# Output-weight remainders on VectorE, one block sum moved ahead of the moments, and tensor-and-scalar forms for 128x1 operations in an attention, experts and SoLU kernel

## The reference, cut to what matters

```python
def _moe_ref(x, domain_probs, w1, w2):
    for e in range(E):                       # 4 experts, 512 -> 1024 -> 512
        h = np.maximum(x @ w1[e], 0.0)
        out += p[:, e:e + 1] * (h @ w2[e])

def _moe2_ref(x, w_in, w_out, g_ln):
    h = x @ w_in                             # 1536 x 512 @ 512 x 1024
    h_max = np.max(h, axis=-1, keepdims=True)
    e = np.exp(h - h_max)
    sm = e / (np.sum(e, axis=-1, keepdims=True) + 1e-09)
    solu = h * sm
    mu = np.mean(solu, axis=-1, keepdims=True)
    var = np.mean((solu - mu) ** 2, axis=-1, keepdims=True)
    ln = (solu - mu) / np.sqrt(var + 1e-06) * g_ln
    return (ln @ w_out).astype(np.float32)   # 1536 x 1024 @ 1024 x 512
```

## Time and profile before

| what | value |
|---|---|
| median of 3 runs | 753.34 us (753.29 to 753.89) |
| the profiled execution's own time | 753.5 us |
| its span, first to last instruction | 751.7 us |
| mean granted clock of PE | 1.000 |
| PE busy | 744.6 us, 99% |
| DVE busy | 525.5 us, 70% |
| POOL busy | 341.0 us, 45% |
| ACT busy | 218.9 us, 29% |

### The profile page before, as it was taken

One profiled execution on the slowest core, in us unless ns is written; L12 is line 12 of the kernel. 1 busy time (PEld: TensorE's weight loads), 2 busy tenths in 40 slices (PEclk: granted clock), 3 DMA queues, 4 the chain that ended last, 5 costly groups with the idle time before them and its releaser, 6 DMA issues. The chain is left out here.

```text
span 751.7 us, 12616 instructions
## 1 busy us (share of the span) xinstructions
PE 744.6 (99%) x3994; PEld 652.9 (87%) x3994; DVE 525.5 (70%) x1042; ACT 218.9 (29%) x414; POOL 341.0 (45%) x326
## 2 busy tenths in 40 slices
PE   9999999999999999999999999999999999999998
PEld 8888899899898998989988898898898877888876
DVE  5677767676666766767666676676767799867772
ACT  5677641111111111111211112111113743433332
POOL 4367546253542535425354253543535974442400
PEclk9999999999999999999999999999999999999999
DMA  9756310100101000010000100000022100000001
GB/s 263 194 142 167 105 31 2 56 29 29 31 26 56 28 28 28 28 56 28 28 28 28 56 28 28 28 28 0 1 112 66 49 0 15 15 29 28 16 28 42
DMA packets 39106, 37.15 MB, mean 49 GB/s; under 512 B 14497, under 2 KB 31905, under 8 KB 39073
## 3 DMA queue, kind: packets, MB, share of 16 engines
q1 hardware_dynamic: 37472, 34.64, 15.0%
q10 hardware_dynamic: 1600, 2.10, 0.8%
HBM read 33.59 MB, written 3.15 MB: 49 GB/s over the span
## 5 line engine op out<-in xcount | busy, mean ns | idle before, releaser
L809 PE MATMUL y_ps<-w2s,hs 128*128 128x512 f32 x1140 | 286.0, 395 | 0.1
L789 PE MATMUL p_ps<-xs,ws 128*128 128x384 f32 x1344 | 255.2, 336 | 0.0
L809 PEld LDWEIGHTS y_ps<-w2s,hs 128*128 128x128 f32 x1140 | 212.4, 188 | 41.0 <-DVE acc L1474 0.6
L789 PEld LDWEIGHTS p_ps<-xs,ws 128*128 128x128 f32 x1344 | 237.6, 188 | 11.0
L1474 DVE SCALAR_TENSOR_TENSOR acc<-y_ps,pr,acc 128x512 f32<-128x512 f32 x178 | 133.0, 748 | 79.6 <-PE y_ps L809 78.6
L1121 ACT ACTIVATE hs<-hs_sum 128x384 fp32r<-128x384 f32 x128 | 67.4, 527 | 353.6 <-DVE hs_sum L1442 238.9
L1461 DVE SCALAR_TENSOR_TENSOR hs<-hs_sum,hs 128x384 fp32r<-128x384 f32 x128 | 93.2, 737 | 4.3 <-ACT hs L1121 2.2
L577 POOL TENSOR_TENSOR ws_sum<-raw_sum 128x256 f32<-128x256 f32 x16 | 11.8, 739 | 146.8 <-PE p_ps L789 146.0
L608 POOL CAST w2s<-raw_sum 128x1024 fp32r<-128x1024 f32 x16 | 16.9, 1056 | 86.1 <-PE y_ps L809 86.1
L1134 ACT ACTIVATE neg_s<-neg_s,row 128x256 f32<-128x256 f32 (+1 forms) x96 | 42.2, 483 | 26.0 <-DVE row L1493 25.9
L1493 DVE CUSTOM_DVE_ANT_0 neg_s<-s_ps,bias 128x256 f32<-128x256 f32 (+1 forms) x96 | 34.3, 399 | 20.2 <-PE s_ps L823 18.1
(11 more groups left out here) (152 smaller groups left out, 971.2 us busy)
## 6 DMA issues: line engine op xcount, KB each, us to landing
raw_sum<-in_w SPq DMA_DIRECT2D x28, 512.0 KB, 3.5
qk<-in_qkW SPq DMA_DIRECT2D x24, 256.0 KB, 3.7
qk<-in_qkW SPq DMA_DIRECT2D x24, 128.0 KB, 4.1
v_sb<-in_v SPq DMA_DIRECT2D x16, 192.0 KB, 3.0
out<-o_sb SPq DMA_DIRECT2D x12, 256.0 KB, 2.0
raw_sum<-in_w ACTq DMA_DIRECT2D x4, 512.0 KB, 7.0
raw_sum<-in_w_in SPq DMA_DIRECT2D x1, 2048.0 KB, 8.0
wout_lo_a_sum<-in_w_out SPq DMA_DIRECT2D x1, 1792.0 KB, 7.6
```

The costliest lines, as they stand in the source:

```text
L789: mm = nc.tensor.matmul(bank, ws[slot][:, w, part, kk, :], xs[:, 2 * bt + kk, x, part, :], start=(kk == 0 and w == 1 and x == 1), stop=(kk ...
L809: mm = nc.tensor.matmul(mixed_at(s, t), hs[bt][:, h, b, tok], w2s[slot][:, w, f, :], start=(f == 0 and h == 1 and w == 1), stop=(f == 1 an ...
```

## The change

- `w_out`: ACT no longer scales chunks 0 to 3 in place. The high parts of all eight chunks are made with the gain as scale, those of chunks 0 to 3 where the scaling stood. POOL's `split_wout` is gone. DVE makes all eight remainders: chunk 0 inside step 31, chunks 1 to 3 behind the last `add_up`s, chunks 4 to 7 one by one between the first block sums.
- `w_in`: POOL makes six remainders instead of five, DVE one instead of two.
- DVE's loop over steps ends one round (four steps) earlier, and that round is written out.
- In the second pair `late_left(1)` stands ahead of `moments(0)`.
- Five 128x1 operations of DVE (`largest`, one in `moments`, two in `normal`) take the form with one tensor and one scalar per partition.

```diff
-    WIN_POOL = 5
+    WIN_POOL = 6
...
-            def split_wout(c):
-                pool.wait_ge(wouthi_ready, c + 1)
-                pool.sem_inc(pool_waited, 1)
-                nc.gpsimd.tensor_tensor(wout_lo(c), wout_raw(c), f32(wout_hi(c)), ALU.subtract).then_inc(wout_ready, 1)
...
             for q in range(2):
-                for c in range(2):
-                    split_wout(2 * q + c)
                 x2_sums(q)
                 x2_los(q)
...
                         if s == 0:
-                            pe.wait_ge(wout_ready, FC // 2)
-                            pe.wait_ge(wout_split, FC // 2)
+                            pe.wait_ge(wout_ready, FC)
...
             def wout_hi_part(c):
-                if c < FC // 2:
-                    act.wait_ge(wout_scaled, c + 1)
-                    nc.scalar.activation(wout_hi(c), wout_raw(c), ACT.Copy).then_inc(wouthi_ready, 1)
-                else:
-                    nc.scalar.activation(wout_hi(c), wout_raw(c), ACT.Copy, scale=gain_sb[:, c:c + 1]
-                                         ).then_inc(wouthi_ready, 1)
-
-            def scale_wout(c):
-                nc.scalar.activation(wout_raw(c), wout_raw(c), ACT.Copy, scale=gain_sb[:, c:c + 1]).then_inc(wout_scaled, 1)
+                nc.scalar.activation(wout_hi(c), wout_raw(c), ACT.Copy, scale=gain_sb[:, c:c + 1]).then_inc(wouthi_ready, 1)
...
             for c in range(FC // 2):
-                scale_wout(c)
+                wout_hi_part(c)
             relu_hi(LAST, 3, 1)
-            for c in range(FC // 2):
-                wout_hi_part(c)
             relu_hi(LAST, 2, 1)
...
                 third_sum(s, i)
+                if isinstance(a, int) and s == LAST:
+                    wout_lo_part(0)
                 add_up(s - 1, 3, 1 - bt, expert, first)
...
             for t in range(4):
                 add_up(LAST, t, 1, E - 1)
-                if t in (0, 2):
-                    win_lo_part(WIN_POOL + t // 2)
+                if t == 1:
+                    win_lo_part(WIN_POOL)
+                if t > 0:
+                    wout_lo_part(t)
...
-                nc.vector.tensor_tensor(st[:, 0:1], st[:, 9:10], st[:, 10:11], ALU.min).then_inc(max_ready, 1)
+                nc.vector.tensor_scalar(st[:, 0:1], st[:, 9:10], st[:, 10:11], None, ALU.min).then_inc(max_ready, 1)
...
-                link(nc.vector.tensor_tensor(st[:, 4:5], st[:, 3:4], st[:, 3:4], ALU.mult))
+                link(nc.vector.tensor_scalar(st[:, 4:5], st[:, 3:4], st[:, 3:4], None, ALU.mult))
...
-                link(nc.vector.scalar_tensor_tensor(st[:, 7:8], st[:, 3:4], -1.0, st[:, 6:7], ALU.mult, ALU.mult))
-                link(nc.vector.scalar_tensor_tensor(st[:, 8:9], mv[:, m, 0:1], -1.0, st[:, 7:8], ALU.mult, ALU.mult))
+                link(nc.vector.tensor_scalar(st[:, 7:8], st[:, 3:4], st[:, 6:7], -1.0, ALU.mult, ALU.mult))
+                link(nc.vector.tensor_scalar(st[:, 8:9], mv[:, m, 0:1], st[:, 7:8], -1.0, ALU.mult, ALU.mult))
...
             def first_pair():
                 wout_lo_part(4)
+                late_left(0)
                 wout_lo_part(5)
-                late_left(0)
+                second_up(0)
                 wout_lo_part(6)
-                second_up(0)
+                third_up(0)
                 wout_lo_part(7)
-                third_up(0)
...
                 solu_part(0)
+                late_left(1)
                 moments(0)
-                late_left(1)
```

More of the change, by code:

```diff
@@ L360, in attention_experts_solu_kernel @@
         winlo_dve = sem("winlo_dve")
-        wout_scaled = sem("wout_scaled")
         wouthi_ready = sem("wouthi_ready")
         wout_ready = sem("wout_ready")
-        wout_split = sem("wout_split")
         p_done = sem("p_done")
@@ L1662, in _, with win_lo_part, wout_lo_part @@
                 attend_wide()
+            def win_lo_part(at):
+                n = WIN_ORDER[at]
+                dve.wait_ge(winhi_ready, at + 1)
+                nc.vector.tensor_tensor(win_lo_at(n), win_sum_at(n), f32(win_hi[:, n]), ALU.subtract
+                                        ).then_inc(winlo_dve, 1)
+            def wout_lo_part(c):
+                if c == 0:
+                    dve.wait_ge(gain_loaded, 16)
+                dve.wait_ge(wouthi_ready, c + 1)
+                nc.vector.scalar_tensor_tensor(wout_lo(c), wout_raw(c), gain_sb[:, c:c + 1], f32(wout_hi(c)),
+                                               ALU.mult, ALU.subtract).then_inc(wout_ready, 1)
             def halve(a, i):
@@ L1688, in _ @@
                 halve(0, i)
-            with dve.Fori(1, STEPS // 4) as a:
+            with dve.Fori(1, STEPS // 4 - 1) as a:
                 for i in range(4):
                     halve(a, i)
[L1693 to L1706, removed]
+            for i in range(4):
+                halve(STEPS // 4 - 1, i)
             for t in range(4):
                 add_up(LAST, t, 1, E - 1)
-                if t in (0, 2):
-                    win_lo_part(WIN_POOL + t // 2)
+                if t == 1:
+                    win_lo_part(WIN_POOL)
+                if t > 0:
+                    wout_lo_part(t)
             def negated(q, n, m, half, other):
```

## The result

The changed kernel takes 755.16 us (median of 16 runs, 754.98 to 755.74), the one before 753.37 (16 runs, 753.21 to 754.01): ratio 1.0024, 95% interval 1.0017 to 1.0031, or +1.8 us. The profiled execution after took 754.98 us with a span of 753.2 at full clock, 1.5 us more than the one before.

What follows compares the result with a forecast made beforehand. PE is busy for 99% of the span, so only its pauses count. +0.37, +2.0 and +1.9, less 1.55, 0.4 and 0.04, give +1.9; taken as +1.8 on 753.5, forecast 755.2 us, range 752.6 to 757.1.

Steps and rivals of the forecast that it cites:

- the signs that it is wrong: late_left ends by 607.7, PE's DVE waits between 600 and 616 under 1 us, or 128x1 minima still reach 1 us.
- the price of the chunks ahead of `third_up`: Pair 0: DVE's remainders wait behind POOL, making PE's product 5 start 2.0 us late and product 3 3.9 in all.
- the order: late_left(1) ahead of moments(0) in pair 1: 0, as the next product gives back 0.3 us; up to 0.4 cost.
- the forms: New 128x1 operations on DVE take 0.147 us without waiting for POOL; 1.5 us off DVE's chain, half reaching PE.
- Its cover: Chunk 0 in step 31: DVE's 1.24 us idle ahead of 593.92 takes in nearly all of the 1.4 us delay.
- what POOL gains: POOL's first half for pair 1 ends at 610.7, not 614.13; PE's 1.67 us pause goes; product 1 at +2.35.
- rival 3: The form changes nothing: 128x1 operations still wait for POOL; +2.7, 756.0 us; chance 0.08.
- The first: Rival 1: at 592.2 POOL's sixth remainder beats relu's, step 31's mix starts 1.5 us later still; +3.3, 756.7 us; chance 0.14.
- The second: Rival 2: chunks 1 to 6 mostly fall between POOL's operations, late_left ready by 607.6; -2.5 us, 750.9; chance 0.12.
- The fourth: Rival 4, partly hidden: one or two waits (chunk 1's 2.2 us, chunk 6's 1.6) fall away; about 753.8 us; chance 0.20.
- what I allowed for the round: DVE's written-out loop round saves register work and a branch: 0, with up to 0.2 us for code that runs once.
- read as in the prediction: Skill's first reading: equal outermost counts, one against one included, take both ports, so new 128x1 forms would wait as before.

Runs made afterwards that it cites:

- The square of four kernels: Changed kernel with old or new 128x1 forms and old or new order of late_left(1): old forms 755.00 (old order), 755.53; new forms 754.76 (old order), 755.16 us.
- the re-placed kernels: Changed kernel with w_out and w_in remainders in new places: 751.43 us; the same with old order and new form for the minimum only: 750.84 us.

## Why the prediction was right

The predicted 755.2 us and the measured 755.16 agree, and the range and the sign were right. So was the mechanism: operations of DVE that stand behind POOL's hold back the block sums, and PE waits for these. None of the signs that it is wrong appeared: `late_left` ended at 608.79, PE's waits on DVE between 600 and 616 us sum to 3.0 us, and the minima took 0.215 us at most. But that the two numbers are 0.04 us apart is luck. In the traces the shift is +1.5 us where the sum gave +1.9, and 0.3 us of that difference are covered by where the two profiled executions lie against their medians. The steps missed by more, and made up for one another: the price of the chunks ahead of `third_up` was too high, that of chunk 7, of the order and of the forms too low.

**Right, step by step.** Chunk 0 takes 2.40 us, as worked out from POOL's fourth remainder. Its cover held: the `add_up` behind it began at 589.75 (589.87 forecast) and DVE was idle 0.79 us ahead of 593.80 all the same. The mix of step 31 starts 0.21 us late (0.37 forecast). The `w_in` remainder and chunk 1 end at 601.60 and 604.41 (601.8 and 604.6). PE then waits for `late_left` of pair 0, later for the third sum; POOL's token remainder is ready for product 1 of pair 1, and `ln_lo`'s pause at tile 1 disappears. That the remainders cost 1.5 us is shown by the kernel that has nothing else but ACT's part and the written-out round.

**Too dear: chunks 3 and 5.** I let chunk 3 stand behind one sum of POOL and chunk 5 until 611.2. Chunk 3 came 0.06 us ahead of POOL's L723 and took 0.73; chunk 5 found POOL between two operations and took 0.74. So `late_left` ended at 608.79 instead of 609.6, PE's wait was 1.25 us instead of 2.0, product 4 had none, and product 3 came 1.6 us late instead of 3.9.

**Too cheap: chunk 7.** The step "what POOL gains" took the pause ahead of product 1 of pair 1 for gone. It changed hands: POOL was ready, but chunk 7 had stood behind POOL until 614.52 and held the fourth sum, for which PE waited 1.32 us. The forecast has POOL's second half for pair 1 (610.6 to 613.5 there, though the sentence calls it the first) in front of chunk 6, until 614.05. In the run chunk 6 met the first half and ended at 611.72, and the second half fell on chunk 7. I had followed the wait at chunk 6 to `third_up` and not the next one to `fourth_up`. Moving this chunk alone won 1.7 us.

**Too cheap: the order.** I put it at 0, with up to 0.4 "when DVE arrives early". DVE did arrive early, by 0.53 us, and for ACT's copy, not for PE's product. The square of four kernels gives 0.4 to 0.5.

**The forms.** That they don't wait for POOL was right, and rival 3 falls: no minimum above 0.215 us, `ln_lo`'s wait gone in the kernel with the forms alone. Their price was wrong. I took 0.147 us from L1779, whose scalar is a constant; in the same trace L1788, a 128x1 operation with a tensor for its scalar, took 0.214 in all its 12 places:

```profile
L1788 DVE TENSOR_SCALAR stats<-mv,stats x12: 214/214/216, 619.8 to 734.8; 128x1 f32<-128x1 f32 x12
```

This row of before was the nearest and I didn't use it. The last chain therefore got 0.2 us longer at tile 10's transposes, not 0.04 shorter. On the kernel before, the forms together are worth -0.66 us.

**The rivals.** The first (POOL wins the tie at 592.2) did not come: relu's remainder started at 591.99 and took 0.54, POOL's sixth waited for it (2.76 for 2.42). The lead was 0.06 us, as thin as I had said. The second, faster because DVE finds gaps, is what the re-placed kernels do. I gave it 750.9 us; with the order and forms of the change it measured 751.43, and the 750.84 of the other kernel, which has the old order and three old forms, are this number by chance. It was a question of places, and with the places of this change the condition (`late_left` ready by 607.6) was missed by 1.2 us. The fourth came in part: of the two waits that it names, chunk 1's was there in full (2.88 us) and chunk 6's was shorter (1.74 us in all), and chunks 3 and 5 had none; chunk 7 took it back.

Not tried: the written-out last round of the loop by itself, and ACT's four dropped scalings by themselves. So no run shows what I allowed for the round (0, up to 0.2 us). Nothing in the traces names it as a cost; the 0.17 us put down to issue ahead of the mix of step 31 may be relu's remainder or this.

## What to carry to other kernels

When two engines keep each other out for whole operations, the price of an operation is its duration and, on top, how long the other engine's operation still runs when it arrives. So place the movable ones next to short operations of the other engine, or where it is idle, and look up in its timeline where its long ones stand: here one remainder of 0.74 us in the wrong place was worth 1.7 us. And after every wait that a change adds, follow the queue behind it to the next thing that the bottleneck waits for, even where the operation that ended its wait until now is known to be early. For a price, take the row whose kinds of operand are the same (constant or tensor for the scalar), not the one whose name is.

## What the runs showed of the hardware

- A 128x1 operation with one tensor and a tensor for its scalar takes 0.214 us (the medians of L1731, L1767, L1774, L1781 and L1782, 12 each, in the changed kernel); with a constant 0.146 (L1765); the old minimum with two tensors 0.159 where it doesn't wait (the least of its 12). Where POOL is idle the new form is thus 0.055 us slower than the old one.
- It doesn't wait for POOL. In the changed kernel five minima, one of them at 655.36 us, ran inside POOL's L735 and took 0.21 us each; the same five took 0.76 to 1.07 in the kernel before. In the kernel with the forms alone the two of pair 0 ran inside POOL's L742, at 613.74 and 614.67, and took 0.21, where they had taken 1.52 and 1.71. The same kind of operation over 1024 columns does wait (1.38 us at most, 0.81 else).

```profile
651.88 4.38 POOL L735 TENSOR_TENSOR x<-x_sum,x 128x768 fp32r<-128x768 f32 x2 [0.20 <-POOL x_sum L726]
...
655.36 0.21 DVE L1731 TENSOR_SCALAR stats<-stats 128x1 f32<-128x1 f32 x1
```

  By the Trainium skill, Advanced Engine Details and Errata, "2x-2p Requirements", the mode that needs both ports wants an even count, or an odd one above one that is equal on both sides. The runs agree with this. They do not agree with VectorE: DVE Perf Modes, "What auto-detection actually checks", in the Trainium skill, if it is read as in the prediction, by which a count of one, being equal on both sides, would do; its words are "outermost non-unit dims", which leave a count of one open. No run has an odd count above one.
- When the two start within 0.1 us of each other, the starts of the rows don't tell who will wait. DVE won with a lead of 0.06 us in two places: chunk 3 at 606.31 against POOL's sum at 606.37 in the changed kernel, and relu's remainder at 591.99 against POOL's at 592.05. But the wide operation of L1783 at 691.66 took 1.38 us, although POOL's sum (L717, 0.74 us) starts at 691.75, and ended 0.55 us after it, as one that had waited.
